# Maxout over expert-sorted rows: y tiles stored densely, gate and token number carried in the rows, output rows scattered

## Chip, cores and metric

The kernel runs on one core of one Trainium2 chip. The metric is device time in microseconds. Before the change the median of three runs is 1018.04 us (1016.11 to 1018.49); the profiled execution took 1017.2 us.

## The reference

Three stages in a row, all in float32. N = 3072 tokens (4 sequences of 768), width 512.

```python
# 1: attention, 8 heads of 64: window of 128 keys and 4 sink keys
a = softmax(where(keep, q @ k.T / 8, -1e9));  x = a @ v      # -> (3072, 512)
# 2: mixture of 8 experts, each token goes to one
logits = x @ w_gate + modality_bias[modality_id];  e = argmax(logits)
gate = softmax(logits)[e]
x = gate * (maximum(x @ w1[e], 0) @ w2[e])                   # 512 -> 1024 -> 512
# 3: Maxout layer
h = maximum(maximum(x @ w1, x @ w2), x @ w3)                 # 512 -> 768
out = h @ w_out                                              # 768 -> 512
```

In these inputs three experts get tokens; sorted by expert they fill 26 tiles of 128 rows, the last of each expert partly.

## The kernel before

All products of the last two stages are made of three float32r matmuls: each operand is split in a high part (ScalarE, a copy with rounding) and a low part (VectorE, original minus high), and `product` sums hi*hi, hi*lo and lo*hi.

**Attention** (up to 235 us) goes over 96 units of one head pair and 128 queries. GpSimd's part is `spread_sinks` and, for each finished sequence, `scatter`: six indirect DMAs that write 128 rows of `x_rows` each to `x_sorted`, at the position `pos` of the token among its expert's rows. `choose_gate` leaves the token's gate in a tile `gate` that stays to the end. Between the loads of q, k and v the SP queue also loads the first expert's weights, the Maxout weights, and zeroes the part of `y_sorted` behind row 3072.

**Tables** (240 to 262 us). From the counts VectorE works out which expert is where: `tab_i` row 0 says from which row of `x_sorted` tile j is read, row 1 whether it needs new weights. SP writes 128 zero rows behind each expert's last row. Between and after these steps VectorE makes `w1_lo`, the first `xT_lo`, and `pos_out`, the row of each token in `y_sorted`, where tile j lies at row 128 j. GpSimd waits for `pos_out_ready` before its loop.

**Expert stage** (257 to 593 us) runs over pairs of tiles, 24.5 us a pair, in one loop with 16 iterations, of which 13 do work. TensorE: `up` (hidden layer of a tile), `turn_h` (transposes), `turn_x` (transposes of the next x tile), `down`. ScalarE: `keep_xT`, `split_w1`, `split_w2`, `keep_h`, `keep_hT`, then `store_y` for both tiles, which issues the store of 128 rows on ScalarE's own queue. VectorE: the same tiles' low parts, and `keep_y`, which copies the result from PSUM to `y`. GpSimd loads the next x tiles (`load_x`). SP loads the second and third expert's weights when the first ones are split.

**Hand-over.** VectorE counts `experts_done` up after the loop; GpSimd waits for all stores (`stored`), and then gathers group 0 and 1 with eight indirect DMAs, one for each 128 tokens, through `pos_out`. A group is four tiles of 128 tokens. Meanwhile VectorE and ScalarE split Maxout weights (`split_m`, six slices of 128 columns; the first two were begun on ScalarE in the attention stage).

**Maxout stage** (611 us to the end), six groups of 67 us each. VectorE multiplies the gathered rows by the gate (`scale_y`); TensorE transposes them into PSUM (`turn_y`, banks `Y_BANK`); ScalarE and VectorE make `yT_hi` and `yT_lo` (`keep_yT`). `maxout(g)` makes 36 matmuls for each of six slices f, three results of 128 columns by 512 tokens, in two sets of banks; ScalarE and VectorE take the maximum, and a set is free for slice f + 2 when `g_kept` says so. `project(g)` makes four output tiles; ScalarE copies each to `o_sb`, and SP stores it to its place in `out`. The next group's tiles are transposed between `maxout` and `project`. A gather of group g + 2 starts when the tiles of group g are transposed.

The hand-over as GpSimd and TensorE see it:

```python
            pool.wait_ge(y_stored, stored)
            ...
            gather(0, 0)
            gather(1, 1)
```

Of the kernel before, what the change touches and what calls it, by code (L numbers as in the profile page):

```python
# [18 lines left out]
def build_program(nc, q_t, k_t, v_p, v_s, dims, n_sink, window, modality_id, w_gate, modality_bias, w1, w2,  # L19
# [25 lines left out]
    Y_BANK = (2, 3, 4, 1)  # L45

    x_sorted = nc.dram_tensor("x_sorted", (E * CAP, DM), F32, kind="Internal").ap()
    y_sorted = nc.dram_tensor("y_sorted", (TMAX * P, DM), F32, kind="Internal").ap()

    ctx = ExitStack()  # L50
    with ctx:
# [11 lines left out]
        pos_out = sb(ctx, "pos_out", [P, NT], I32)  # L63
        gate = sb(ctx, "gate", [P, NT])
        tab_i = sb(ctx, "tab_i", [P, 2, TW], I32)
# [7 lines left out]
        shift = sb(ctx, "shift", [P, E])  # L73
        moved = sb(ctx, "moved", [P, NT, E])
        pos_y = sb(ctx, "pos_y", [P, NT])
        onehots = sb(ctx, "onehots", [P, B, QT, E])
        zeros = sb(ctx, "zeros", [P, DM])
# [39 lines left out]
        x_rows = sb(one, "x_rows", [P, 2, QT, DM])  # L117
# [21 lines left out]
        near_i = sb(one, "near_i", [P, 1], I32)  # L139
        all_keys = sb(one, "all_keys", [P, S])  # L140
# [12 lines left out]

        cnt = sb(one, "cnt", [P, E])
# [16 lines left out]
        tab_f = sb(one, "tab_f", [P, 2, TW])  # L171
# [15 lines left out]
        y = [sb(two, f"y{i}", [P, DM]) for i in range(2)]  # L187
# [7 lines left out]
        yr = [sb(three, f"yr{i}", [P, GT, DM]) for i in range(2)]  # L195
# [43 lines left out]
        pos_out_ready, y_zeroed = sem("pos_out_ready"), sem("y_zeroed")  # L239
# [12 lines left out]
        results_there, o_free = sem("results_there"), sem("o_free")  # L252

        gathered = [sem(f"gathered{i}") for i in range(2)]
        m_hi_made, m_lo_made = sem("m_hi_made"), sem("m_lo_made")
        gated, y_turned, yT_hi_made, yT_lo_made = sem("gated"), sem("y_turned"), sem("yT_hi_made"), sem("yT_lo_made")
# [28 lines left out]
        def _(sp):  # L285
# [26 lines left out]
            assert len(between) == PAIRS - 2  # L312

            for g in range(2, PAIRS):
                sp.wait_ge(qk_free, g - 1)
                load_qk(g)
                sp.wait_ge(values_done, QT * (g - 1))
                load_v(g)
                dst, src, loaded = between[g - 2]
                sp.dma_start(dst, src).then_inc(loaded, 16)  # L320

            sp.wait_ge(counts_ready, 1)
            for e in range(E):
# [1152 lines left out]
```

## Time and profile before

| | before |
|---|---|
| median of three runs | 1018.04 us |
| profiled execution, its own time | 1017.2 us |
| its span, first to last instruction | 1015.6 us |
| TensorE busy | 945.2 us, 93% of the span |
| VectorE, ScalarE, GpSimd busy | 408.6, 310.2, 95.3 us |
| mean granted TensorE clock | 0.975 of full |
| one Maxout group, from one group's transposes to the next | 67.06 us |
| pitch of the matmuls of 512 columns there | 0.227 us |
| TensorE starts up(0,1), the second tile's first product | 265.60 us |
| y_sorted, one store, issue to landing | 2.0 us |

Times inside the profile count from the start of the span. An engine's name with a q behind it (ACTq, POOLq) is its sequencer, and the DMAs that it issues. The chain is the chain of work that ended last, followed back from the last instruction. The clock column tells the share of TensorE's full clock that was granted in a stretch.

### The profile page before, as it was taken

The numbers are of one execution on the slowest core, as the hardware profiler recorded it, in microseconds if no ns is written. First come the engines' busy times: TensorE is split into PE (matmuls) and PEld (weight loads), VectorE is DVE, ScalarE is ACT, GpSimd is POOL, SyncE is SP. The second block draws the span as 40 slices with busy tenths as digits, with TensorE's granted clock in tenths as the row PEclk, the third lists the DMA queues.
The fourth block names the chain that finished last, engine by engine and source line by source line (L and its number), as shares of the span: only waits on it lengthen the run. The fifth ranks groups of instructions, "written<-read, shape, count | busy, mean of one in ns | idle before, by whom it ended". The sixth has DMA issues, their size and how long they took to land.

```text
span 1015.6 us, 15686 instructions
## 1 busy us (share of the span) xinstructions
PE 945.2 (93%) x5166; PEld 757.7 (75%) x5166; DVE 408.6 (40%) x1308; ACT 310.2 (31%) x755; POOL 95.3 (9%) x175
## 2 busy tenths in 40 slices
PE   3999999991899999899999939999999999999998
PEld 2777776771788888678888737888888888888887
DVE  4778786866622222442222465312313223123120
ACT  2677676763311111321111333121211211112111
POOL 2111313132000000000000031010100100000000
PEclk9999999995899999999999979999999999999999
DMA  4455646534511111331111031020110200100001
GB/s 102 141 180 171 215 163 225 173 123 157 207 42 45 48 41 41 114 116 49 41 41 41 31 94 51 1 84 1 38 45 0 72 10 0 41 1 11 32 1 42
DMA packets 35987, 76.99 MB, mean 76 GB/s; under 512 B 7520, under 2 KB 9568, under 8 KB 35936
## 3 DMA queue, kind: packets, MB, share of 16 engines
q1 hardware_dynamic: 22048, 49.55, 14.3%
q0 software_dynamic: 6080, 19.93, 6.4%
q10 hardware_dynamic: 7808, 6.87, 2.1%
q8 instruction: 27, 0.44, 0.2%
q14 instruction: 24, 0.20, 0.1%
HBM read 52.74 MB, written 23.59 MB: 75 GB/s over the span
## 4 chain that ended last, share of the span: by engine, by line
PE 92%; DVE 4%; DMA 1%; issue 1%; ACT 1%; POOL 0%; DVEq 0%; ACTq 0%; POOLq 0%
PE bank L627 23%; PE bank L629 22%; PE bank L628 22%; PE bank L482 5%; PE bank L524 5%; PE bank L494 5%; PE bank L501 2%; PE bank L654 2%; PE bank L513 2%; PE bank L698 1%; PE bank L622 1%; DMA limits_i<-in_window 1%; DVE w_lo L1265 0%; DVE masked L991 0%; DVE w_lo L1311 0%
## 5 line engine op out<-in xcount | busy, mean ns | idle before, releaser
L629 PE MATMUL bank<-yT_hi,m_lo 128*128 128x512 f32 x432 | 168.3, 390 | 0.0
L756 ACT ACTIVATE probs<-masked,row_min 128x264 f32<-128x264 f32 (+1 forms) x192 | 93.4, 487 | 77.6 <-DVE row_min L991 77.6
L627 PE MATMUL bank<-yT_hi,m_hi_b 128*128 128x512 f32 x288 | 112.2, 390 | 0.0
L628 PE MATMUL bank<-yT_lo,m_hi_b 128*128 128x512 f32 x288 | 112.2, 390 | 0.0
L1397 DVE TENSOR_TENSOR b_sb<-bank,a_sb 128x512 f32<-128x512 f32 x36 | 24.9, 691 | 187.7 <-PE bank L629 187.7
L629 PEld LDWEIGHTS bank<-yT_hi,m_lo 128*128 128x128 f32 x432 | 81.1, 188 | 16.8
L627 PE MATMUL bank<-w_hi,xT_hi 128*128 128x512 f32 x208 | 84.7, 407 | 9.3 <-DVE w_lo L1265 5.0
L627 PE MATMUL bank<-w_hi,hT_hi 128*128 128x512 f32 x208 | 83.3, 400 | 5.1 <-DVE w_lo L1265 5.1
L915 ACT ACTIVATE gT_hi<-g_sb 128x512 fp32r<-128x512 f32 x36 | 22.8, 632 | 200.1 <-DVE g_sb L1400 200.1
L629 PE MATMUL bank<-w_hi,xT_lo 128*128 128x512 f32 x208 | 83.0, 399 | 0.0
L628 PE MATMUL bank<-w_lo,xT_hi 128*128 128x512 f32 x208 | 82.7, 398 | 0.0
L991 DVE CUSTOM_DVE_ANT_0 masked<-bank,masks 128x264 f32<-128x264 f32 (+1 forms) x192 | 70.5, 405 | 28.1 <-PE bank L482 27.1
L629 PE MATMUL bank<-w_hi,hT_lo 128*128 128x512 f32 x208 | 81.6, 393 | 0.0
L628 PE MATMUL bank<-w_lo,hT_hi 128*128 128x512 f32 x208 | 81.6, 392 | 0.0
L482 PE MATMUL bank<-kT,qT 64*128 64x264 f32 (+2 forms) x384 | 67.0, 428 | 12.0 <-issue 11.6
L869 ACT ACTIVATE xT_hi<-bank 128x512 fp32r<-128x512 f32 x27 | 16.6, 614 | 185.8 <-PE bank L622 185.8
L494 PE MATMUL bank<-ident,probs 128*128 128x128 f32 x352 | 61.1, 294 | 4.2 <-ACT probs L756 4.2
L628 PEld LDWEIGHTS bank<-yT_lo,m_hi_b 128*128 128x128 f32 x288 | 54.1, 188 | 11.2
L627 PEld LDWEIGHTS bank<-yT_hi,m_hi_b 128*128 128x128 f32 x288 | 54.1, 188 | 11.1
L524 PE MATMUL bank<-pT,v_in 128*64 128x128 f32 x704 | 60.4, 289 | 0.0
L524 PEld LDWEIGHTS bank<-pT,v_in 128*64 128x64 f32 x704 | 36.9, 137 | 29.5 <-issue 21.7
L627 PE MATMUL bank<-yT_hi,m_hi_a 128*128 128x512 f32 x144 | 56.2, 390 | 1.4 <-DVE yT_lo L1376 1.4
(189 smaller groups left out, 1562.5 us busy)
## 6 DMA issues: line engine op xcount, KB each, us to landing
w_sb<-in_moe_w SPq DMA_DIRECT2D x4, 2048.0 KB, 9.2
xr<-x_sorted POOLq DMA_DIRECT2D x28, 256.0 KB, 3.0
y_sorted<-y ACTq DMA_DIRECT2D x26, 256.0 KB, 2.0
kT<-in_k_t SPq DMA_DIRECT2D x16, 400.0 KB, 4.1
qT<-in_q_t SPq DMA_DIRECT2D x16, 384.0 KB, 3.4
v_in<-in_v_p SPq DMA_DIRECT2D x16, 384.0 KB, 2.9
out<-o_sb SPq DMA_DIRECT2D x24, 256.0 KB, 2.0
m_sb<-in_moe_w SPq DMA_DIRECT2D x6, 768.0 KB, 6.3
```

The costliest lines, as they stand in the source:

```text
L482: pe.matmul(bank[2 * (n % 2) + hd][:, 0:win_of(t)], qT[g % 2][rows, t * P:(t + 1) * P], kT[g % 2][rows, win_at(t):win_at(t) + win_of(t)], ...
L494: mm = pe.transpose(bank[(4, 7)[n % 2]][:, col:col + P], probs[n % 2][:, hd, at:at + P], ident[:, :])
L501: pe.matmul(bank[5][:, 0:PW], oT[n % 2][:, :], to_rows[:, n // QT % PPB, :], start=True, stop=True).then_inc(rows_ready, 1)
L513: pe.matmul(bank[6][:, 0:P], v_sink[g % 2][:, :], sink_cols[n % 2][:, :, :].rearrange("p a c -> p (a c)"), start=True, stop=False, skip_gr ...
L524: mm = pe.matmul(bank[6][D * hd:D * hd + D, 0:P], v_in[g % 2][:, tile, D * hd:D * hd + D], pT[n % 2][:, col:col + P], start=t < 2 and w == ...
L627: pe.matmul(psum, a_hi, b_hi, start=first, stop=False)
L628: pe.matmul(psum, a_hi, b_lo, start=False, stop=False)
L629: return pe.matmul(psum, a_lo, b_hi, start=False, stop=last)
L756: last = act.activation(probs[n % 2][:, hd, 0:win_of(t)], masked[n % 2][:, hd, 0:win_of(t)], ACT.Exp, bias=row_min[:, n % 2, hd:hd + 1], s ...
L915: act.activation(gT_hi[:, f, :], g_sb[:, f % 2, :], ACT.Copy).then_inc(gT_hi_made, 1)
L991: dve.tensor_tensor_reduce(out=masked[n % 2][:, hd, 0:win_of(t)], in0=bank[2 * (n % 2) + hd][:, 0:win_of(t)], in1=masks[:, min(t, 2), 0:wi ...
L1397: dve.tensor_tensor(b_sb[:, f % 2, :], bank[b0 + 1][:, :], a_sb[:, f % 2, :], ALU.max).then_inc(b_kept, 1)
```

## The change

- `keep_y` multiplies by the gate as it takes the result out of PSUM, so `scale_y` goes.
- Every row of `x_sorted` and `y_sorted` grows from 512 to 514 numbers; the last two are the gate and the token number. They are put into `x_rows` by `choose_gate` and by an iota of GpSimd, travel with the row, and come into `y` by a small load of its own, `load_meta`.
- `store_y` writes tile j at the row where the expert's rows really begin, so that experts follow each other without gaps; the zero rows at an expert's end are overwritten by the next expert's first tile, and therefore a store waits for the one before it. `tab_i` gets a third row with these starts, ready with `y_rows_ready`, for which ScalarE and GpSimd wait before their loops. `pos_out` and the zeroing of `y_sorted` go.
- The Maxout stage takes the rows in sorted order, 512 to a group, by plain loads on SP (`load_y`). Group 0 is loaded as soon as 12 tiles are stored, into `yr_first`, which no longer shares memory with expert tiles, and transposed into banks 4, 5, 6, 1.
- Output tiles are written by 24 indirect DMAs on GpSimd, to the rows that the token numbers name.
- At the hand-over `keep_yT(0)` comes first on ScalarE and behind one slice of `split_m` on VectorE; before, two and four slices came first.

```diff
-            for c in range(2):
-                at = slice((NT + c * (TMAX - NT) // 2) * P, (NT + (c + 1) * (TMAX - NT) // 2) * P)
-                between.append((y_sorted[at, :].rearrange("(t p) d -> p t d", p=P),
-                                zeros[:, None, :].broadcast_to([P, (TMAX - NT) // 2, DM]), y_zeroed))
...
-            def store(g):
-                for t in range(GT):
-                    sp.wait_ge(o_kept, GT * g + t + 2)
-                    sp.dma_start(out[bass.ds((GT * g + t) * P, P), :], o_sb[:, t, :]).then_inc(out_stored, 16)
...
+            def load_y(g):
+                sp.dma_start(yr[g % 2][:, :, :], y_sorted[g * GN:(g + 1) * GN, 0:DM].rearrange("(t p) d -> p t d", p=P)
+                             ).then_inc(y_loaded[g % 2], 16)
+
+            sp.wait_ge(y_stored, 16 * FIRST_TILES + 1)
+            load_y(0)
+            sp.wait_ge(results_there, 1)
+            sp.wait_ge(experts_done, 1)
+            load_y(1)
+            sp.dma_start(token[:, :, :], y_sorted[0:N, DM:XW].bitcast(I32).rearrange("(t p) o -> p t o", p=P)
+                         ).then_inc(token_loaded, 16)
+            for g in range(2, G):
+
+                sp.wait_ge(y_turned, GT * (g - 1))
+                load_y(g)
...
+            def name_tokens(b):
+
+                if b >= 2:
+                    pool.wait_ge(x_scattered, 16 * QT * (b - 1))
+                step(pool.iota(x_rows[:, b % 2, :, TOKEN].bitcast(I32), pattern=[[P, QT]], base=b * S, channel_multiplier=1))
...
+            def load_meta(j, par):
+                row = pool.value_load(tab_i[0:1, 0, bass.ds(j, 1)], min_val=0, max_val=E * CAP - P)
+                pool.dma_start(y[par][:, DM:XW],
+                               x_sorted[bass.ds(row, P), DM:XW]).then_inc(meta_loaded[par], 16)
...
+                    pool.wait_ge(y_stored, 32 * i + 1)
+                    for par in range(2):
+                        load_meta(2 * i + par, par)
...
-            gather(0, 0)
-            gather(1, 1)
...
+            pool.wait_ge(token_loaded, 16)
+            for g in range(G):
                 for t in range(GT):
+                    j = GT * g + t
+                    pool.wait_ge(o_kept, j + 2)
                     pool.indirect_dma_start(
+                        out=out[:, :], out_offset=bass.IndirectOffsetOnAxis(ap=token[:, j, TOKEN - DM:TOKEN - DM + 1], axis=0),
+                        in_=o_sb[:, t, :], in_offset=None).then_inc(out_stored, 16)
+                if g < G - 1:
+                    pool.wait_ge(out_stored, 16 * GT * (g + 1))
+                    pool.sem_inc(o_free, 1)
...
+            def turn_y(g, par, uses, last_g):
+                pe.wait_ge(y_loaded[par], 16 * uses)
+                banks = Y_BANK if last_g is not None else FIRST_BANK
                 for t in range(GT):
-                    pe.wait_ge(gated, GT * g + t + 1)
...
             def store_y(j, par):
+                row = act.value_load(tab_i[0:1, 2, bass.ds(j, 1)], min_val=0, max_val=N)
                 act.wait_ge(y_kept, j + 2)
-                act.dma_start(y_sorted[bass.ds(j * P, P), :], y[par][:, :]).then_inc(y_stored, 16)
+
+                act.wait_ge(y_stored, 16 * j + 1)
+                act.dma_start(y_sorted[bass.ds(row, P), :], y[par][:, :]).then_inc(y_stored, 16)
...
-            act.wait_ge(y_zeroed, 32)
             keep_xT(0, 0)
+            act.wait_ge(y_rows_ready, 1)
             with act.Fori(0, TMAX // 2) as i:
...
             act.wait_ge(experts_done, 1)
-            for f in range(2, 4):
-                split_m(f)
-            keep_yT(0)
-            for f in range(4, F3C):
+            keep_yT(0, FIRST_BANK)
+            for f in range(2, F3C):
                 split_m(f)
...
-                dve.wait_ge(y_stored, 32 * i + 1)
-                dve.tensor_copy(y[par][:, :], bank[out_bank][:, :]).then_inc(y_kept, 1)
+                dve.wait_ge(meta_loaded[par], 16 * i + 16)
+                dve.tensor_scalar(y[par][:, 0:DM], bank[out_bank][:, :], y[par][:, GATE:GATE + 1], None, ALU.mult
+                                  ).then_inc(y_kept, 1)
...
-            step(dve.tensor_scalar(shift[:, :], base[:, :], -1.0, None, ALU.mult))
-            step(dve.tensor_tensor(moved[:, :, :], onehots[:, :, :, :].rearrange("p b t e -> p (b t) e"),
-                                   shift[:, None, :].broadcast_to([P, NT, E]), ALU.mult))
-            step(dve.tensor_reduce(pos_y[:, :], moved[:, :, :], AX.X, ALU.add))
-            dve.tensor_tensor(pos_out[:, :], pos_y[:, :], pos[:, :], ALU.add).then_inc(pos_out_ready, 1)
+            step(dve.tensor_tensor(less_t[:, :, :], less[:, :, :], cnt[:, None, :].broadcast_to([P, E, E]), ALU.mult))
+            step(dve.tensor_reduce(first_y[:, :], less_t[:, :, :], AX.X, ALU.add))
+            step(dve.tensor_scalar(base[:, :], t_start[:, :], float(-P), None, ALU.mult))
+            step(dve.tensor_tensor(base[:, :], base[:, :], first_y[:, :], ALU.add))
+            step(dve.tensor_scalar(tm_b[:, :, :], cl, float(P), None, ALU.mult))
+            step(dve.tensor_tensor(tm_b[:, :, :], tm_b[:, :, :], by_expert(base), ALU.add))
+            step(dve.tensor_tensor(tm_b[:, :, :], tm_b[:, :, :], tm_a[:, :, :], ALU.mult))
+            step(dve.tensor_reduce(tab_f[:, 2, :], tm_b[:, :, :], AX.X, ALU.add))
+            dve.tensor_copy(tab_i[:, 2, :], tab_f[:, 2, :]).then_inc(y_rows_ready, 1)
...
-            for f in range(4):
-                split_m(f)
-            scale_y(0, 0, 0)
-            keep_yT(0)
-            for f in range(4, F3C):
+            split_m(0)
+            keep_yT(0, FIRST_BANK)
+            for f in range(1, F3C):
                 split_m(f)
```

## Rows read from the trace of the kernel before

**Rows 1.** Waits of TensorE from 240 us: line, releaser, total us, times, longest.
```profile
PE bank L698 <- DVE yr L1369: 13.3, 1, 13.3
...
PE bank L627 <- DVE w_lo L1265: 10.1, 4, 2.6
```

**Rows 2.** Chain that ended last, at the hand-over: start us, us, what.
```profile
592.98 0.70 DVE y L1305
...
593.86 2.03 DMA y_sorted<-y
...
596.76 1.51 POOL yr L460
...
602.13 3.53 DMA yr<-y_sorted,pos_out
...
611.32 0.50 PE bank L627
```

**Rows 3.** Timeline at the hand-over: start us, us, what [idle before it].
```profile
591.82 2.37 ACTq L883 DMA_DIRECT2D y_sorted<-y  x2
...
594.90 3.70 DVE L1362 TENSOR_TENSOR m_lo<-m_sb,m_hi_a 128x512 fp32r<-128x512 f32 x6 [1.23 <-issue]
596.20 3.23 ACT L833 ACTIVATE m_hi_b<-m_sb 128x512 fp32r<-128x512 f32 x6 [7.50 <-issue]
```

**Rows 4.** Timeline of ScalarE and VectorE at group 1's tiles.
```profile
661.87 2.04 ACT L909 ACTIVATE yT_hi<-bank 128x512 fp32r<-128x512 f32 x4
...
662.61 2.47 DVE L1376 TENSOR_TENSOR yT_lo<-bank,yT_hi 128x512 fp32r<-128x512 f32 x4
```

**Rows 5.** Windows: us, busy and count of PE, PEld, DVE, ACT, POOL; clock, DMA.
```profile
592.97:596.79 3.82, 0.00 (x0) 0.00 (x0) 2.58 (x5) 0.59 (x2) 0.03 (x1) 1.00 0.30 110
...
606.23:610.40 4.17, 3.67 (x16) 3.27 (x16) 3.20 (x6) 2.25 (x4) 2.02 (x3) 0.50 0.70 199
610.50:611.30 0.80, 0.00 (x0) 0.00 (x0) 0.69 (x1) 0.80 (x3) 0.62 (x1) 1.00 0.02 5
```

**Rows 6.** Windows in the expert loop, around TensorE's wait for w2_lo.
```profile
586.00:588.00 2.00, 0.75 (x3) 0.68 (x4) 2.00 (x2) 2.00 (x3) 0.00 (x0) 1.00 0.00 0
```

**Rows 7.** The last output tile (timeline), and the tile out.
```profile
1012.20 0.60 ACT L930 ACTIVATE o_sb<-bank 128x512 f32<-128x512 f32 x1 [3.48 <-PE bank L629]
...
L342 SPq DMA_DIRECT2D out<-o_sb x24: 332/332/372, 667.3 to 1013.0; - x24
...
DMA to landing us min/median/max: 2.0/2.0/3.9
```

**Rows 8.** Indirect DMAs: yr (640 to 730), x_sorted, and GpSimd's timeline.
```profile
DMA to landing us min/median/max: 3.3/3.5/4.4
...
L418 POOL DMA_INDIRECT x_sorted<-x_rows,pos x6: 960/961/1007, 237.4 to 243.8; - x6
...
248.00 0.59 POOL L434 DMA_DIRECT2D xr<-x_sorted  x1 [3.22 <-DMA x_sorted<-x_rows,pos]
```

**Rows 9.** Timeline, last table steps and start of the expert stage.
```profile
246.63 0.44 DVE L1239 TENSOR_REDUCE tab_f<-tm_b 128x34 f32<-128x272 f32 x1
...
260.05 0.18 DVE L1337 TENSOR_TENSOR pos_out<-pos_y,pos 128x24 int32<-128x24 f32 x1
...
263.05 0.60 ACT L869 ACTIVATE xT_hi<-bank 128x512 fp32r<-128x512 f32 x1 [9.40 <-PE bank L622]
...
264.30 0.54 POOL L441 DMA_DIRECT2D xr<-x_sorted  x1 [1.37 <-issue]
```

**Rows 10.** DMA issues: KB, us to landing; ScalarE's timeline over a pair's end.
```profile
y_sorted<-y ACTq DMA_DIRECT2D x26, 256.0 KB, 2.0
...
mod_i<-in_moe_modality_id ACTq DMA_DIRECT2D x1, 24.0 KB, 7.9
...
279.88 5.70 ACTq L883 DMA_DIRECT2D y_sorted<-y  x2
288.42 0.60 ACT L869 ACTIVATE xT_hi<-bank 128x512 fp32r<-128x512 f32 x1 [14.19 <-PE bank L622]
```

More of the change, by code:

```diff
@@ L62, in build_program @@
         pos = sb(ctx, "pos", [P, NT], I32)
-        pos_out = sb(ctx, "pos_out", [P, NT], I32)
-        gate = sb(ctx, "gate", [P, NT])
-        tab_i = sb(ctx, "tab_i", [P, 2, TW], I32)
+        token = sb(ctx, "token", [P, NT, XW - DM], I32)
+        tab_i = sb(ctx, "tab_i", [P, 3, TW], I32)
         rank_i = sb(ctx, "rank_i", [P, E], I32)
@@ L139, in build_program @@
         near_i = sb(one, "near_i", [P, 1], I32)
+        spare = sb(one, "spare", [P, 1792])
+        zeros = sb(one, "zeros", [P, XW])
         all_keys = sb(one, "all_keys", [P, S])
@@ L152, in build_program @@
         wide.close()
+        first_y = sb(one, "first_y", [P, E])
         cnt = sb(one, "cnt", [P, E])
@@ L186, in build_program @@
         hT_lo = [sb(two, f"hT_lo{i}", [P, F], F32R) for i in range(2)]
-        y = [sb(two, f"y{i}", [P, DM]) for i in range(2)]
+        y = [sb(two, f"y{i}", [P, XW]) for i in range(2)]
+        yr_first = sb(two, "yr_first", [P, GT, DM])
         two.close()
@@ L194, in build_program @@
         mo_hi = sb(three, "mo_hi", [P, F3C, DM], F32R)
-        yr = [sb(three, f"yr{i}", [P, GT, DM]) for i in range(2)]
+        yr = [yr_first, sb(three, "yr_second", [P, GT, DM])]
         yT_hi = sb(three, "yT_hi", [P, KC, GN], F32R)
@@ L697, in turn_y @@
                     for c in range(KC):
-                        mm = pe.transpose(bank[Y_BANK[t]][:, c * P:(c + 1) * P], yr[par][:, t, c * P:(c + 1) * P], ident[:, :])
+                        mm = pe.transpose(bank[banks[t]][:, c * P:(c + 1) * P], yr[par][:, t, c * P:(c + 1) * P], ident[:, :])
                     mm.then_inc(y_turned, 1)
@@ L903, in _, with keep_yT @@
                         store_y(2 * i + par, par)
-            def keep_yT(g):
+            def keep_yT(g, banks):
                 for t in range(GT):
@@ L1363, in split_m, with keep_yT @@
                 last.then_inc(m_lo_made, 1)
-            def scale_y(g, par, i):
-                for t in range(GT):
-                    if t == 0:
-                        dve.wait_ge(gathered[par], 16 * GT * (i + 1))
-                    dve.tensor_scalar(yr[par][:, t, :], yr[par][:, t, :], gate[:, bass.ds(GT * g + t, 1)], None,
-                                      ALU.mult).then_inc(gated, 1)
-            def keep_yT(g):
+            def keep_yT(g, banks):
                 for t in range(GT):
@@ L1387, in _, with group @@
             dve.tensor_tensor(mo_lo[:, :, :], mo_sb[:, :, :], mo_hi[:, :, :].bitcast(F32), ALU.subtract).then_inc(m_lo_made, 1)
-            def group(g, par, i, last=False):
+            def group(g, last=False):
                 for f in range(F3C):
@@ L1403, in group @@
                                       ).then_inc(gT_lo_made, 1)
-                    if f == F3C - 3 and not last:
-                        scale_y(g + 1, 1 - par, i + par)
                 if not last:
-                    keep_yT(g + 1)
-            with dve.Fori(0, G // 2 - 1) as i:
-                group(2 * i, 0, i)
-                group(2 * i + 1, 1, i)
-            group(G - 2, 0, G // 2 - 1)
-            group(G - 1, 1, G // 2 - 1, last=True)
+                    keep_yT(g + 1, Y_BANK)
+            with dve.Fori(0, G - 1) as g:
+                group(g)
+            group(G - 1, last=True)
 _INS = ["n_sink", "window", "moe_modality_id", "moe_w_gate", "moe_modality_bias", "moe_w1", "moe_w2",
```

76 lines of the change are left out of this document (33 added, 43 removed).

## The prediction

> **What bounds the kernel now.** I read the waits of TensorE from 240 us on first [rows 1]. The reader is to see how few they are. After the attention stage the matrix engine waits for results in only a handful of places, and the largest single one, 13.3 us before the transposes of line 698, is the hand-over from the expert stage to the Maxout stage. Everywhere else the time is set by the number of matmuls, which this change leaves alone. So the change can win about what that hand-over costs, and lose only where it makes a new wait.
>
> The chain that ended last, followed through the hand-over [rows 2], says what the 13.3 us are made of. The last expert matmul has ended when VectorE copies y at 592.98 (to 593.67), the last y tile is stored (landed at 595.89), GpSimd starts the first of four indirect gathers at 596.76, and the fourth, started at 602.13, lands at 605.66. Then come the scaling by the gate, the 16 transposes (from 606.23, 3.67 us [rows 5]), one ScalarE copy and the last VectorE subtraction; the first Maxout matmul starts at 611.32. From the end of the last expert matmul to it: 18.3 us.
>
> The timeline of the same stretch [rows 3] shows what the other engines would be ready for. VectorE has left the expert loop at 594.90, ScalarE at 596.20. Both then do splits that the transposed tiles don't depend on.
>
> **The change at the hand-over.** Group 0's four y tiles now come by a plain load issued on SP once 12 tiles are stored, out of the 26 of this run. It waits behind the expert weights in SP's queue, but those are all issued 150 us before the hand-over, so the data is there. TensorE's 16 transposes need nothing else (banks 4, 5, 6, 1 are already read) and follow the last expert matmul at about 593; at the full clock they take half of their 3.67 us, so they end near 595. That they come early is no gain in itself, since the copies set the end: ScalarE does its first yT_hi copy where it now does its first split, 596.20. VectorE does split_m(0), three subtractions at 3.70/6 = 0.62 us, from 594.90 to 596.75, and then the four yT_lo. In the steady state four such copies take ScalarE 2.04 us and four subtractions take VectorE 2.47 us [rows 4]. With the first yT_hi ready at about 596.8, VectorE ends at 596.85 + 2.47 = 599.3 and the first Maxout matmul starts at 599.35. That is 611.32 - 599.35 = 12.0 us earlier. The gathers, the scaling by the gate and the landing of the last store lie off the path.
>
> ScalarE's start could move. A store now waits for the store before it: the one issued at 591.82 lands 2.0 us later [rows 3, 10], that is at 593.85, where the second store was issued anyway. I charge 0.1 us, so 11.9. From below VectorE's own order holds: it can't finish before 594.90 + 1.85 + 2.47 = 599.2, a gain of 12.1. From above, ScalarE spends 2.0 us between its last store and its first split, all of it issue; twice that gives a gain of 9.9.
>
> Is something late next? After 599.3 VectorE owes five splits (5 x 1.85) and the split of mo (about six chunks of 0.62, 3.7), so it is free at 612.3, and g_sb of the first f is kept at about 613.7. TensorE wants it for the third f, 72 matmuls at the steady pitch of 0.227 us after 599.35, at 615.7. It fits, with 2 us to spare.
>
> **The clock.** TensorE now stops twice instead of once. In the trace its clock is at the full level (2.4 GHz) for the first 3.8 us of idleness and at half (1.2 GHz) when it restarts at 606.23, and is at the full level again from 610.5 [rows 5]; the price fell on transposes, inside the wait. In the expert loop a wait of 2.6 us left the level at 1.00 [rows 1, 6]. After the change the idle stretch behind the early transposes is about 594.8 to 599.35, 4.5 us, longer than the one that kept the level and about as long as the one that had lost it. If the level falls, the first Maxout matmuls run at half rate, at most for the 4.2 us of [rows 5], which costs half of that, 2.1 us, and nothing if it holds. I take 1.7, since part of the half-rate stretch can lie in the idle time.
>
> A rule bears on this. In rows 5 nothing but transposes ran between 606.23 and 609.9, and the level rose right after them: transposes count. The Trainium skill, TensorE: Matmul & The Clock Gate, Part 4 (PE-mode transpose), says the opposite, that a transpose doesn't count as busy in the same way. By that rule the early transposes would not shorten the pause, the fall would be certain, and the cost the full 2.1 us in place of 1.7; by this case's rows it is less. It is a rival below.
>
> **The end.** Output rows leave by an indirect DMA on GpSimd instead of a plain store on SP. The last o_sb is kept at 1012.80, SP issues at 1013.0 and the rows land 2.0 us later at 1015.0, 0.6 before the end of the span [rows 7]. Now GpSimd takes 0.3 us to start, as between its gathers, and an indirect DMA lands 3.5 us after its issue in the quiet Maxout stage (3.3 to 4.4); at the end of the attention stage GpSimd waited 3.22 us for a scatter of such rows beyond the 0.96 us of issuing it [rows 8]. So 1012.80 + 0.3 + 3.5 = 1016.6 in place of 1015.0: +1.6 us. Bounds: +0.3 if it lands as a plain store does, 2.0 us after its start (nothing makes it faster than that), and +2.7 with the 4.4. The skill's page DMA: Bandwidth & Descriptors, Anatomy of one DMA, fits 2.0 us plus bytes over 436e3 for a DMA from GpSimd, an estimate of 2.6 us for 256 KB, by which the tail would be +0.7. The other 20 scatters are hidden: an output tile comes every 4.1 us (18 matmuls), a scatter occupies GpSimd for 1.0 us, and o_sb is wanted again only a group (67 us) later.
>
> **The start of the expert stage.** Four VectorE steps (259.07 to 260.23) become nine: four on the tile table, of which three like the one of 0.44 us, two of 64 elements and three short ones, together about 2.9 us instead of 1.16. y_rows_ready thus comes at 261.98, and ScalarE now waits for it before its loop. Behind that wait stand three register loads and the copy of the second x tile, which ran at 263.05 [rows 9]. A register load and the issue around it took GpSimd 1.37 us [rows 9]. If ScalarE's three overlap, it is ready at 263.5; if they don't, at 262.0 + 4.1 = 266.1, which is 3 us late. TensorE wants that tile's xT_lo only when up(0,1) starts, at 265.60, and VectorE makes it in 0.7 us after ScalarE's copy, by 264.4 in the trace, so 1.2 us of delay is free. Cost: 0 to 1.9 us; I take 0.3, as ScalarE's loads are short where it leaves the loop (2.0 us for everything, rows 3). VectorE's own extra 1.75 us is covered by its wait for the same copy; GpSimd's next x load comes 1.75 us later, with 8 us to spare before the transposes that read it.
>
> **Edits at nothing.** The metadata loads (one per tile, 8 bytes a row) are queued on GpSimd behind the next x loads; they are issued some 5 us into a pair, and needed when down(i,0) ends, 15 us later. Value for price: the modality numbers, 24 KB in pieces of the same 8 bytes, landed in 7.9 us [rows 10], and that is also the size of the token load, which is wanted 45 us after it is issued. Without that cover either would cost up to 7.9 us once (the token load) or the part past 15 us in each of 13 pairs. Multiplying y by the gate on its way out of PSUM has the shape of a VectorE operation that takes 0.69 us with an immediate factor, the same as the copy it replaces. The iota in the attention stage (at most 0.2 us, four times) lies in GpSimd's waits of over 2 us a unit. Rows of 2,056 bytes instead of 2,048 add 0.4% to hidden transfers. The zeroing of y_sorted and the four scalings in every group go; both were hidden, so they give nothing.
>
> **Sum.** -11.9 (hand-over) + 1.7 (clock) + 1.6 (last scatter) + 0.3 (entry) = -8.3 us. Against the profiled execution's 1017.2 us that is 1008.9. It lies 0.8 below the median of the runs, 1018.04; I lay the difference on the middle of the two, 1017.6, and get 1009.3. A measurement of this kernel can't tell changes within about 0.3% (3 us) from none.
>
> **Rivals.**
> - The clock holds through the second pause. For it: a 2.6 us wait did no harm and the early transposes cut the pause. Against: 4.5 us is nearer to the pause that lost it. 1009.3 - 1.7 = 1007.6 us. Chance 0.25.
> - Transposes don't count (the skill's rule above): a fall for certain and its full price, 1009.7 us. Against it stands the rise at 610.5. Chance 0.06.
> - A new wait takes part of the place: ScalarE reaches the first yT_hi up to 2 us later than 596.2 because its longer loop code has to be left, or the entry to the expert loop costs its 1.9 us. Each gives 1010.5 to 1011.5, both together 1013.3. Chance 0.12.
> - The load of group 0 is not early after all (behind SP's queue), so that its landing takes the place of the gathers: issue at 595.9, four tiles in about 6 us, the transposes at 602 and the matmuls at 607, 4 us of gain against 1.6 of tail and no change to be measured, 1015.5. Against it: SP's queue is empty 150 us earlier. Chance 0.03.
> - Slower: the wait in store_y. ScalarE now stands still until the store before has landed. It issues a pair's first store at 279.88 and is next wanted at 288.42 [rows 10]. With a landing of 2.0 us nothing happens; if the rows of 2,056 bytes, not aligned in memory, took more than 8.5 us, each further us would be paid in all 13 pairs. From 9.4 us on the kernel is slower by over 0.3%; at 10 us it takes 1009 + 13 x 1.5 = 1029 us. Only the size of the landing decides, and the slowest y store or gather around here took 4.4 us. Chance 0.04.
>
> **How the numbers follow.** The forecast (gain, clock falls) has 0.50, its own range 1008 to 1010.5. Faster by over 0.3%, that is below 1014.6 to 1015: 0.50 + 0.25 + 0.06 + 0.12 = 0.93 less 0.01 for a bad sum of upper ends: 0.92. Within 0.3%: 0.03 and that 0.01, 0.04. Slower: 0.04. The range takes in the rival with the clock held and a short tail (1007.6 - 1.3, 1006.3) and most of the new waits, up to 1012.5.
>
> **What the profile will show.** Right: the wait of line 698's successor before group 0 gone; 16 transposes straight behind the last expert matmul; the first Maxout matmul 6.4 us after it, not 18.3; a granted clock of 0.50 for up to 4 us there; the last scatter landing about 3.8 us after the last o_sb; the pairs of the expert loop as long as before (24.5 us). Wrong: TensorE waiting for y_loaded; VectorE waiting for the metadata; an entry to the expert loop later than 265.5 at the second tile; stores that land after more than 8 us.

## The result, and the profile after

| | before | after |
|---|---|---|
| median | 1017.09 us (4 runs, 1016.11 to 1018.49) | 1024.48 us (4 runs, 1023.57 to 1026.02) |
| profiled execution, its own time | 1017.2 us | 1023.57 us |
| its span | 1015.6 us | 1021.7 us |

The ratio is 1.0069 (95% interval 1.0051 to 1.0087): slower, 15 us above the forecast. In the two spans the 6.1 us divide so (my sums, from the start of one row to the start of another; a pair is the time from one `turn_h` to the next but one, two tiles):

| stretch | before | after | difference | forecast |
|---|---|---|---|---|
| start to first `up` | 257.27 | 258.83 | +1.6 | 0 |
| first `up` to first `turn_h` | 13.77 | 14.40 | +0.6 | +0.3 |
| the two pairs around the first change of expert | 57.90 | 62.49 | +4.6 | 0 |
| ten other pairs | 247.94 | 249.04 | +1.1 | 0 |
| last pair, to the last copy of y | 16.10 | 17.60 | +1.5 | 0 |
| hand-over, to the first Maxout matmul | 18.34 | 6.57 | -11.8 | -11.9 |
| Maxout stage, to the last `o_sb` | 400.88 | 402.28 | +1.4 | +1.7 |
| last `o_sb` to the end of the span | 3.4 | 10.5 | +7.1 | +1.6 |

The waits of TensorE from 240 us (line, releaser, total us, times, longest) answer to [rows 1]:

```profile
PE bank L640 <- DMA xr<-x_sorted: 16.1, 1, 16.1
PE bank L645 <- DVE w_lo L1285: 10.1, 4, 2.6
PE bank L645 <- DVE xT_lo L1307: 6.9, 3, 4.7
PE bank L645 <- DVE yT_lo L1394: 4.9, 1, 4.9
```

The 13.3 us before line 698 are gone. In their place stand 4.9 us for the first `yT_lo`, as forecast (4.5), and, not forecast, one wait of 4.7 us for an `xT_lo`: a new stall inside the expert loop.

The chain at the hand-over (start us, us, what), against [rows 2]:

```profile
602.36 0.76 DVE y L1325
603.37 2.41 DMA y_sorted<-y
605.78 0.60 ACT yT_hi L931
606.40 2.49 DVE yT_lo L1394 x4
608.93 0.79 PE bank L645
```

Behind the last y copy stand 2.7 us until ScalarE starts its first copy, this copy, and four subtractions: no gather, no scaling, no transpose. The chain puts 2.4 of the 2.7 us down to the landing of the last y store. That is an inference which the code doesn't bear out: ScalarE waits for the store before the last one, and for the last one only GpSimd waits. From the start of the y copy to the start of that ScalarE copy are 3.4 us here and 3.3 in e4_no_wait below, where ScalarE waits for no store; the prediction had 3.2, for leaving the loop.

The windows (columns as in [rows 5]), over the second half of the expert stage's last weight change, the pause, and the first Maxout matmuls:

```profile
594.00:599.00 5.00, 3.87 (x11) 3.08 (x12) 4.55 (x5) 2.57 (x3) 0.00 (x0) 0.66 0.00 0
...
606.00:608.50 2.50, 0.00 (x0) 0.00 (x0) 2.28 (x5) 2.50 (x6) 0.00 (x0) 1.00 0.23 17
608.50:611.90 3.40, 2.97 (x7) 2.39 (x8) 3.40 (x7) 3.40 (x8) 0.00 (x0) 0.50 1.05 300
612.00:614.00 2.00, 2.00 (x10) 1.67 (x9) 2.00 (x4) 2.00 (x5) 0.00 (x0) 1.00 0.89 131
```

The clock fell to its lower level at the first Maxout matmul, for the 3.4 us of the window, as the likeliest case had it. It also fell in the last pair (0.66 on average over 594 to 599), where [rows 6] had shown it unmoved.

The end, in the timeline, against [rows 7]:

```profile
1011.21 0.60 ACT L952 ACTIVATE o_sb<-bank 128x512 f32<-128x512 f32 x1 [3.48 <-PE bank L647]
1012.08 0.97 POOL L484 DMA_INDIRECT out<-o_sb,token  x1 [3.11 <-ACT o_sb L952]
```

The scatter starts 0.27 us after the copy and lands 2.7 us after its start (the median of the 24), at 1014.8. But the span goes on to 1021.7. What runs in those 7 us shows in the instructions of the program's last line, which every engine executes (duration ns, min/median/max, then first and last start):

```profile
L55 POOLq DRAIN  x1: 9611/9611/9611, 1011.8 to 1011.8; - x1
L55 SPq COMPARE_BRANCH  x1: 38/38/38, 1014.8 to 1014.8; - x1
L55 SPq DRAIN  x1: 7/7/7, 1015.0 to 1015.0; - x1
L55 SPq EVENT_SEMAPHORE  x1: 17/17/17, 1021.6 to 1021.6; - x1
```

SyncE has seen the last scatter land at 1014.8 and would be through at 1015. GpSimd's closing drain, 9.6 us from 1011.8 on, is what the other engines meet at 1021.5. In the kernel before, the same instruction took longer and cost nothing, since GpSimd's work ended with the gathers, 219 us before the end:

```profile
L51 POOLq DRAIN  x1: 11484/11484/11484, 796.5 to 796.5; - x1
```

In the view of waits SyncE's last 6.7 us are put down to another engine, which had long been done: the releaser named there is an inference, and the long instruction beside it is the cause.

The stall in the expert loop, ScalarE's timeline around 440 us, after:

```profile
431.62 3.90 ACT L870 ACTIVATE w_hi<-w_sb 128x1024 fp32r<-128x1024 f32 x4 [4.72 <-PE bank L647]
438.78 8.33 ACTq L905 DMA_DIRECT2D y_sorted<-y  x2
450.41 0.60 ACT L888 ACTIVATE xT_hi<-bank 128x512 fp32r<-128x512 f32 x1 [14.90 <-DMA y_sorted<-y]
```

and before:

```profile
437.51 4.00 ACTq L883 DMA_DIRECT2D y_sorted<-y  x2
444.42 0.60 ACT L869 ACTIVATE xT_hi<-bank 128x512 fp32r<-128x512 f32 x1 [10.04 <-PE bank L622]
```

Before, the pair's two stores were issued within 4.0 us and ScalarE waited for TensorE. After, the second store's issue ends 8.3 us after the first began, and the next `xT_hi` comes 11.6 us after the first store in place of 6.9. The first store is in flight while the next expert's weights arrive (two DMAs of 2 MB, on SP's queue from 421.66 on; the second is issued at 437.4 and lands at 447.8). It is the slowest y store of this trace, and it isn't slower than it was; the landings of all y stores, after and then before:

```profile
DMA to landing us min/median/max: 2.4/2.8/7.8
```

```profile
DMA to landing us min/median/max: 2.0/2.0/7.9
```

So the new wait makes the stall, and no new slowness of the store.

The table's 4.6 us for these two pairs are the net of two things. The pair with the stall takes 35.27 us, 6.2 more than before: 4.7 of waiting, and a fall of the clock behind it, at 451. The pair ahead of it takes 27.21 us, 1.6 less than before, since a fall of the clock that the trace of before has at 416 is missing here. Where the same stall meets a trace with that fall, in e1_sp_out below, the two pairs take 63.8 us, 5.9 more than before.

### The profile page after: what moved, and what is told of

The parts are those of the page before. It is cut to its first block, busy times and chain, and to the rows that moved or that the text cites. A ratio compares the mean times of both kernels' runs of the same rounds, so it can differ in the third digit from the quotient of the medians.

```text
span 1021.7 us, 15881 instructions
## 1 busy us (share of the span) xinstructions
PE 948.0 (93%) x5166; PEld 757.9 (74%) x5166; DVE 401.5 (39%) x1289; ACT 309.6 (30%) x755; POOL 108.5 (11%) x205
## 4 chain that ended last, share of the span: by engine, by line
PE 89%; DVE 4%; DMA 2%; issue 2%; ACT 1%; POOL 1%; ACTq 0%; POOLq 0%; DVEq 0%
PE bank L645 22%; PE bank L647 22%; PE bank L646 21%; PE bank L500 5%; PE bank L542 5%; PE bank L512 5%; PE bank L519 2%; PE bank L672 2%; PE bank L531 2%; DMA y_sorted<-y 1%; PE bank L640 1%; PE bank L717 1%; DMA limits_i<-in_window 1%; DVE w_lo L1285 1%; POOL x_sorted L430 1%
## 5 line engine op out<-in xcount | busy, mean ns | idle before, releaser
L645 PE MATMUL bank<-w_hi,xT_hi 128*128 128x512 f32 x208 | 85.1, 409 | 11.9 <-DVE xT_lo L1307 6.9
L500 PE MATMUL bank<-kT,qT 64*128 64x264 f32 (+2 forms) x384 | 67.3, 430 | 11.9 <-issue 11.6
L484 POOL DMA_INDIRECT out<-o_sb,token x24 | 23.3, 971 | 411.4 <-ACT o_sb L952 411.4
## 6 DMA issues: line engine op xcount, KB each, us to landing
xr<-x_sorted POOLq DMA_DIRECT2D x28, 256.0 KB, 3.0
```

Source lines behind the costliest of these rows:

```text
L484: pool.indirect_dma_start(out=out[:, :], out_offset=bass.IndirectOffsetOnAxis(ap=token[:, j, TOKEN - DM:TOKEN - DM + 1], axis=0), in_=o_sb ...
L500: pe.matmul(bank[2 * (n % 2) + hd][:, 0:win_of(t)], qT[g % 2][rows, t * P:(t + 1) * P], kT[g % 2][rows, win_at(t):win_at(t) + win_of(t)], ...
L645: pe.matmul(psum, a_hi, b_hi, start=first, stop=False)
```

## The experiments

Each is compared with the kernel before on the same chip. Two questions had the most at stake: what the last 7 us are, and what the expert loop lost.

**e1_sp_out: the output stores back on SP.**

```diff
+                for t in range(GT):
+                    sp.wait_ge(o_kept, GT * g + t + 2)
+                    sp.dma_start(out[(GT * g + t) * P:(GT * g + t + 1) * P, :], o_sb[:, t, :]).then_inc(out_stored, 16)
...
-                    pool.indirect_dma_start(
-                        out=out[:, :], out_offset=bass.IndirectOffsetOnAxis(ap=token[:, j, TOKEN - DM:TOKEN - DM + 1], axis=0),
-                        in_=o_sb[:, t, :], in_offset=None).then_inc(out_stored, 16)
```

> The changed kernel with its 24 output tiles stored by plain DMAs on SP, as before the change, in sorted order (so output rows stand in another order; all arithmetic is done). Theory A (GpSimd's closing DRAIN, which ran from 1011.85 to 1021.46 us in the changed kernel and from 796.5 to 808.0, hidden, in the kernel before, is exposed because GpSimd now issues the last DMA): the span ends about 2.8 us after the last o_sb instead of 9.9, 7 us less than the changed kernel, about 1017.4 us. Rival B (the scatters slow the Maxout stage, or land late): the drain stays as it is or the gain is spread over the six groups; B by landing alone would give back 14.8 - 15.0 = nothing, under 1 us.

Measured: 1017.58 us, ratio 1.0003 (0.9987 to 1.0019), against 1.0069 with the scatters. From the last `o_sb` (1010.61) to the end of the span (1013.5) are 2.9 us instead of 10.5. The drain is still there, just ahead of the Maxout stage and 400 us before the end:

```profile
L55 POOLq DRAIN  x1: 6441/6441/6441, 605.9 to 605.9; - x1
```

So the 7 us at the end belong to GpSimd being the last to work, and not to the landing of the rows.

**e2_late_plain: the kernel before, with one plain 256 KB store on GpSimd after the last output tile.**

```diff
+            pool.wait_ge(o_kept, NT + 1)
+            pool.dma_start(late_out[:, :], o_sb[:, GT - 1, :]).then_inc(late, 16)
```

> The kernel before the change, plus one plain 256 KB store that GpSimd issues after the last output tile is kept, into a scratch tensor. Theory A (any late DMA of GpSimd pulls the drain to the end): slower than the kernel before by about 6 to 7 us, 1023 to 1024 us, with a DRAIN of 8 to 10 us at the end of GpSimd's program. Rival B (it is peculiar to indirect DMAs): slower by 1 to 2 us only, for the landing of 3.0 in place of 2.0 us.

Measured: 1023.18 us, ratio 1.0072 (1.0055 to 1.0088). One plain store is enough to turn the kernel before into one as slow as the changed one. Its last `o_sb` is at 1012.74, and the last line's instructions are:

```profile
L53 POOLq DRAIN  x1: 6974/6974/6974, 1013.6 to 1013.6; - x1
L53 SPq DRAIN  x1: 7/7/7, 1016.6 to 1016.6; - x1
```

SyncE is done at 1016.6, the span ends at 1020.8. An indirect DMA is not needed for the price.

**e8_drain_early: the changed kernel with a drain of GpSimd before its last two scatters.**

```diff
+                    if j == NT - 2:
+                        pool.drain()
                     pool.wait_ge(o_kept, j + 2)
```

> The changed kernel with one explicit drain of GpSimd put before its last two scatters. In the first experiment the closing DRAIN took 6.4 us although GpSimd's last DMA lay some 20 us behind it. Theory A (a drain costs this fixed time whenever it is taken): the closing DRAIN still takes over 8 us and the time stays at 1024. Rival B (it clears up after all software DMAs since the last drain, and an early one leaves little): the closing DRAIN shrinks and the time falls by up to 5 us, to 1019.

Measured: 1023.07 us, ratio 1.0043 (1.0028 to 1.0058). The trace is of the fastest of the four runs, 1018.58 us (the others: 1023.00 to 1023.57), so only its rows at the end are used here, not its time. The closing drain shrank to 3.9 us, and ends with the landing of the last scatter. But the inserted one took its place:

```profile
L484 POOLq DRAIN  x1: 9447/9447/9447, 1002.1 to 1002.1; - x1
...
L55 POOLq DRAIN  x1: 3856/3856/3856, 1012.6 to 1012.6; - x1
```

The last two scatters, due at 1006.5 and 1010.5 by the pitch of 4.08 us, started at 1012.32 and 1013.60. So the long drain was paid once here, by whichever drain came first, and it should be free where GpSimd is idle for 9 us; e9_drain_group tests that.

**e4_no_wait: tiles of y at row 128 j, no wait for the store before.**

```diff
-                act.wait_ge(y_stored, 16 * j + 1)
...
-            step(dve.tensor_reduce(tab_f[:, 2, :], tm_b[:, :, :], AX.X, ALU.add))
+            step(dve.tensor_scalar(tab_f[:, 2, :], tile_no[:, :], float(P), None, ALU.mult))
```

> The changed kernel with each y tile stored at row 128 j, so that stores don't overlap and ScalarE doesn't wait for the store before; the register load of the row is kept. The Maxout stage then works on the first 24 stored tiles, padding included, and output tiles are scattered to consecutive rows, so the output is another one; the amount of work is the same. Theory A (the wait for the landing costs 4.7 us once): 4 to 5 us less than the changed kernel, about 1019.5. Rival B (it is the register load or ScalarE's longer loop): less than 1 us less.

Measured: 1015.67 us, ratio 0.9992 (0.9979 to 1.0006). The twelve intervals sum to 305.91 us, against 311.53 after and 305.84 before: the two pairs at the change of expert take 28.85 and 28.90 (27.21 and 35.28 after), the others, but for the last with its change of expert, 24.51 to 24.60 (24.63 to 24.69). A landing is as long as it was (2.4/2.7/7.8 us min/median/max), but nobody waits for it:

```profile
438.08 3.98 ACTq L904 DMA_DIRECT2D y_sorted<-y  x2
444.63 0.60 ACT L889 ACTIVATE xT_hi<-bank 128x512 fp32r<-128x512 f32 x1 [9.73 <-PE bank L641]
```

**e3_pool_store: the ordered stores on GpSimd, each landing waited for.**

```diff
+            def store_y(j, par):
+                row = pool.value_load(tab_i[0:1, 2, bass.ds(j, 1)], min_val=0, max_val=N)
+                pool.wait_ge(y_kept, j + 2)
+                pool.dma_start(y_sorted[bass.ds(row, P), :], y[par][:, :]).then_inc(y_stored, 16)
+                pool.wait_ge(y_stored, 16 * j + 16)
```

> The changed kernel with the ordered y stores issued, and waited for, by GpSimd instead of ScalarE, so that ScalarE never stands still for a landing and needs no row register. Theory A (the 9.4 us lost in the expert stage are 4.7 from the one store that met the second expert's weight load while ScalarE stood still, some 1 us from 0.1 a pair, 2.2 at the entry, 1.5 from a clock fall): 5 to 6 us less than the changed kernel, about 1018.5 us, and no wait of TensorE for xT_lo at the change of expert. Rival B (the wider rows or the metadata loads make the stage longer, whoever issues): the same time as the changed kernel, 1024.

Measured: 1018.59 us, ratio 1.0021 (1.0008 to 1.0034). The ordinary pairs fell to 24.47 us and the pairs of the change to 28.83 and 28.88, but the pair after the change took 26.6, because the wait for the landing now held GpSimd's next x load:

```profile
PE bank L646 <- DMA xr<-x_sorted: 16.8, 2, 14.9
```

Two waits, the first of 14.9 us at the entry, the other of 1.9. The stall had moved, and was smaller.

**e7_pool_store2: as e3_pool_store, with the second store's landing waited for only after the next x loads.**

```diff
+                if par:
+                    pool.wait_ge(y_stored, 16 * j)
+                pool.dma_start(y_sorted[bass.ds(row, P), :], y[par][:, :]).then_inc(y_stored, 16)
...
+                    with pool.If(i > 0):
+                        pool.wait_ge(y_stored, 32 * i)
```

> The full computation. GpSimd issues the y stores, as in the third experiment, but waits for a pair's last landing only behind the next x loads, so that the load of the x tile after a change of expert isn't late (it cost 1.9 us there). Theory A: the stage takes as long as before the change, 2 us less than the third experiment, about 1016.5 us, level with the kernel before. Rival B (GpSimd's program is too full, its loads are late anyway): 1018.5 again.

Measured: 1014.98 us, ratio 0.9957 (0.9942 to 0.9971); the whole computation, and faster than before. The same slow landing is there, in GpSimd's timeline, and delays nothing:

```profile
438.32 0.55 POOL L466 DMA_DIRECT2D y_sorted<-y  x1 [23.27 <-DVE y L1324]
447.15 0.55 POOL L466 DMA_DIRECT2D y_sorted<-y  x1 [8.29 <-DMA y_sorted<-y]
448.89 0.54 POOL L453 DMA_DIRECT2D xr<-x_sorted  x1 [1.19 <-issue]
```

The twelve intervals sum to 305.22 us, 6.3 less than after. 26 loads of metadata and the multiplication by the gate are in these 24.46 us pairs, so they cost nothing.

**e6_row64: rows of 528 numbers, 2,112 bytes (33 x 64), the changed kernel otherwise.**

```diff
-    XW = DM + 2
+    XW = DM + 16
```

> The changed kernel with rows of 528 numbers (2112 bytes, a multiple of 64) in place of 514 (2056): 16 numbers of metadata instead of 2. Rival B (rows that begin off a multiple of 64 bytes land more slowly): a y store lands in 2.0 to 2.2 us again instead of 2.8, and GpSimd waits 3.2 us for the last scatter of the attention stage instead of 4.4 to 6.1; the time falls by 1 to 3 us against the changed kernel (1024.5). Theory A (the row width hardly matters, the order of the stores does): landings as in the changed kernel and the same time within 1.5 us.

Measured: 1023.95 us, ratio 1.0043 (1.0029 to 1.0057). The DMA issues (KB each, median us to landing), of the changed kernel and of this one:

```profile
y_sorted<-y ACTq DMA_DIRECT2D x26, 257.0 KB, 2.8
```

```profile
y_sorted<-y ACTq DMA_DIRECT2D x26, 264.0 KB, 2.1
```

More bytes, and 0.7 us less: the row length was behind the slower landing, and behind the longer wait for the last x scatter too (2.96 us here, 4.4 to 6.1 in the ten traces with rows of 2,056 bytes, 3.22 in [rows 8]). The slowest landing stayed (7.6 us), and with it the stall (36.15 us for that pair). So the alignment is real, and isn't what made the kernel slow.

**e5_both: the edits of e1_sp_out and e4_no_wait together.**

> The changed kernel with both edits of the first two experiments on it: plain output stores on SP in sorted order, and y tiles stored at row 128 j with no wait for the store before (so the output is another one; the work is the same). Theory A (the closing drain and the ordered store are all that the forecast missed): the forecast's own time, 1009.3 us, between 1007.5 and 1011; the two gains of 6.9 and 8.8 us add up only in part, since about 1.5 us of the second was a clock fall that some executions have and others don't. Rival B (the rest of the change costs something more that these two hid): above 1012.

Measured: 1007.66 us (6 runs, 1005.76 to 1011.65), ratio 0.9892 (0.9874 to 0.9911). With plain output stores the forecast's 1.6 us for the last scatter fall away too, so the forecast for this kernel is -8.3 - 1.6 = -9.9 us, a ratio of 0.9903: inside the interval. Without the two faults the change is worth what the forecast gave it.

**e9_drain_group and e11_after_drain_group: one drain ahead of the last group**, where GpSimd is idle for 52 us, in e7_pool_store2 and in the changed kernel.

```diff
+                    if j == NT - GT:
+                        pool.drain()
                     pool.wait_ge(o_kept, j + 2)
```

> The full computation, e7_pool_store2 with one drain of GpSimd ahead of the last group of Maxout, where e7's GpSimd stood idle for tens of us. Theory (the closing drain costs what GpSimd's transfers since its last drain have left to clear away): the closing drain falls from 9.8 us to about 4, as in e8_drain_early, and since this drain stands in idle time it holds no scatter: the tail after the last o_sb falls from about 10.5 to 5 us, and the time is 4 to 6 us below e7's ratio of 0.9957, so about 0.990 to 0.992 of before. Rival (a drain costs its full length wherever the last transfer is near): closing drain still near 9 us, time as e7, ratio 0.996. A third: the early drain reaches into the last group and holds its first scatters, which shows as later rows of o_sb in the last group and a ratio near 1.

> The full computation, the changed kernel with one drain of GpSimd ahead of the last group of Maxout and nothing else. Theory: the tail falls from 9.7 to about 5 us and nothing else moves, so some 4.5 us below the changed kernel's 1024.5: about 1020, ratio near 1.002 to 1.003. Rival (the closing drain costs its full length again): 1024, ratio 1.007.

Measured: e9_drain_group 1008.54 us, ratio 0.9893 (0.9876 to 0.9909); e11_after_drain_group 1016.19 us, ratio 0.9971 (0.9958 to 0.9985). Both gained more than expected. Of e9_drain_group the two drains, and the last scatters in GpSimd's timeline:

```profile
L495 POOLq DRAIN  x1: 8237/8237/8237, 941.9 to 941.9; - x1
...
L55 POOLq DRAIN  x1: 3153/3153/3153, 1004.1 to 1004.1; - x1
```

```profile
992.10 0.97 POOL L497 DMA_INDIRECT out<-o_sb,token  x1 [52.07 <-ACT o_sb L953]
996.18 0.97 POOL L497 DMA_INDIRECT out<-o_sb,token  x1 [3.11 <-ACT o_sb L953]
1000.26 0.97 POOL L497 DMA_INDIRECT out<-o_sb,token  x1 [3.11 <-ACT o_sb L953]
1004.34 0.97 POOL L497 DMA_INDIRECT out<-o_sb,token  x1 [3.11 <-ACT o_sb L953]
```

The closing drain now ends at 1007.3, within 0.3 us of the landing of the last scatter (1004.34 + 2.7); no scatter is late. From the last `o_sb` to the end are 4.0 us in both kernels. That is 6.5 us less than after, and it is the price of the undrained end. Between the spans of the changed kernel and e11_after_drain_group (1021.7 and 1013.3) lie 8.4 us: these 6.5, and 2.1 by which the first `up` happened to start earlier (256.77 against 258.83), less 0.2 of small things. By the two ratios the gain is 10 us, but the kernel before took 1019.48 us in this round and 1017.09 in the first one, so ratios of the two rounds don't compare to better than some 2 us. What the traces show of the drain is the 6.5.

**e10_split_early: e9_drain_group, with VectorE's first `split_m` ahead of the expert loop.**

```diff
+            split_m(0)
 
             with dve.Fori(0, TMAX // 2) as i:
...
-            split_m(0)
             keep_yT(0, FIRST_BANK)
```

> The full computation, e9_drain_group with the three subtractions of the first Maxout matrix (m_lo of f = 0) moved from after the expert loop on VectorE to before it. Theory: the hand-over from the last y copy to the first turn_y loses about 1.9 us (three subtractions of about 0.64 us), and the clock either falls as before or not: ratio 0.2 to 0.4 per cent below e9's. Rival (PE waits there for the rows of y_sorted, loaded back, and not for m_lo): hand-over unchanged, time as e9's. A third: the early subtractions wait for the Maxout weights and delay the first xT split, which shows as a later first up.

Measured: 1007.54 us, ratio 0.9881 (0.9865 to 0.9898); against e9_drain_group the intervals overlap, but the trace shows the gain. The hand-over falls from 6.27 to 5.03 us, 1.2 and not 1.9, since another thing is late next, ScalarE's first copy:

```profile
597.21 2.07 ACT L932 ACTIVATE yT_hi<-bank 128x512 fp32r<-128x512 f32 x4 [7.76 <-DVEq L1390]
597.84 2.48 DVE L1397 TENSOR_TENSOR yT_lo<-bank,yT_hi 128x512 fp32r<-128x512 f32 x4 [1.74 <-ACT yT_hi L932]
```

ScalarE waits for VectorE to have left its loop (`experts_done`), 1.9 us after the start of the last y copy. The Maxout stage takes 402.53 us, no less than with the longer pause: the clock still falls.

## Why the prediction was wrong

**The hand-over: right, size and reason.** -11.8 us, forecast -11.9. The first Maxout matmul starts 6.6 us after the last y copy, and it waits for the four `yT_lo`, in the order that was worked out.

**The clock at the first Maxout matmul: right.** +1.4 us, forecast +1.7; in the eleven traces of the changed kernel and its variants the Maxout stage takes 402.3 to 402.8 us, against 400.88. The rival in which the clock holds is refuted, and in e10_split_early a fall came behind a pause of 3.3 us too. The rival in which transposes don't count has the fall as well; its full price of 2.1 us was not reached in any of the eleven, but whether transposes count could not be told from these runs.

**The end: this step failed.** The prediction put it as "1012.80 + 0.3 + 3.5 = 1016.6 in place of 1015.0: +1.6 us". The landing was in fact shorter, 2.7 us. By the Trainium skill, DMA: Bandwidth & Descriptors, Anatomy of one DMA, the estimate was 2.6 us, and the trace agrees. (The two bounds are 0.2 too high by their own terms: 1012.80 + 0.3 + 2.0 and + 4.4 give +0.1 and +2.5.) What failed is the silent step behind it, that the span ends when the last rows have landed. It was so only as long as GpSimd's drain was over before. Moving the last DMA to GpSimd put its closing drain at the end of the path, 5.5 us more than was charged. The row was in the trace of before, 11.5 us long at 796.5, and wasn't priced because nothing waited for it. e1_sp_out, e2_late_plain and e11_after_drain_group each show it alone: without it, with it in the other kernel, and paid early.

**The wait in `store_y`: this step failed.** The prediction charged it 0.1 us at the hand-over, and made it a rival only if the landing took more than 8.5 us in all 13 pairs. No y store took that long. The slowest landed in 7.8 us, and the wait cost 4.7 us there, with a fall of the clock behind it 6.2. Two things were wrong. The 8.5 us were read from one ordinary pair, as the time from the first store to the next `xT_hi`; at the change of expert this time is 6.9 us before. And the landing isn't all that must fit into it: the second store is issued only behind it, and from there to `xT_hi` pass 3.8 us. 7.8 + 3.8 - 6.9 = 4.7 us, which is the wait that TensorE shows. In the other ten pairs the wait cost 0.11 us each, 1.1 us together, where the prediction had said that nothing happens. [rows 10] gave the median landing, 2.0 us, and the text took 4.4 us for the slowest around; that same trace has a y store of 7.9 us, at 437.51, and a wait meets the slowest. e4_no_wait takes both costs away by itself (305.91 us), and e7_pool_store2 does it with the wait kept, on an engine with time to spare.

**The entry: right.** From the first `up` to the first `turn_h` the six traces in which ScalarE doesn't wait for `y_rows_ready` (before, and the kernels whose stores are on GpSimd among them) take 13.73 to 14.27 us, 13.95 on average, the seven in which it does 14.14 to 14.42, 14.36 on average: 0.4 us, forecast 0.3. The pair of traces in the table above gives 0.6, and chance is in it.

**Edits at nothing: right.** The metadata and token loads, the multiplication by the gate (0.75 us where the copy took 0.70) and the zero rows stood beside pairs of 24.46 us in e7_pool_store2, no longer than before (24.49 to 24.60). Rows of 2,056 bytes were not only 0.4% longer: they land 0.7 us later. It is hidden.

**The profiled execution of before was a lucky one in the last pair.** It shows 16.10 us from the last `turn_h` to the last y copy; each of the other twelve traces, e2_late_plain among them, whose expert stage is that of before, shows 17.4 to 17.8. [rows 6] was read as "a wait of 2.6 us left the level at 1.00". In the other traces that same wait was followed by a fall, worth 1.5 us. The reading was partial besides: the 10.1 us of [rows 1] are four such waits, and behind two of them the clock of that same trace did fall, at 416 and 433. The window around the second, before:

```profile
430.00:436.00 6.00, 3.44 (x9) 2.48 (x8) 4.43 (x4) 3.90 (x4) 0.00 (x0) 0.74 0.00 0
```

Over all 13 traces 38 of the 52 waits of 2.5 to 2.6 us have such a fall, by their place in the program 10, 13, 3 and 12 of 13. So of the +6.1 us in the spans the 1.5 us in the last pair are no effect of the change, and no error of the forecast; the 1.6 us by which the pair ahead of the stall is shorter aren't either, and the two cancel.

**What is left.** The forecast was 14.4 us below the span of after (1015.6 - 8.3 = 1007.3 against 1021.7): 5.5 the end, 4.6 the two pairs at the change of expert (6.2 the stall, less the 1.6 just named), 1.1 the other pairs, 1.5 the clock in the last pair, 0.3 the entry, -0.2 the hand-over and the clock together, and 1.6 in the first `up` starting later. The last one stays open: in the traces with the changed tables that start lies anywhere between 256.0 and 258.8 us. Of the 1.6 us 1.2 lie in the attention stage: the last x scatter starts at 245.01 us after and at 243.79 before, and in the thirteen traces anywhere from 243.3 to 245.0. From there on the chain of the trace after runs through the 6.1 us of waiting for that scatter, whose slower landing (e6_row64) may have made the rest; that wasn't separated.

## What to carry to other kernels

Before the last DMA of a kernel is moved to another engine, look at what that engine's closing instructions cost in the trace of before, hidden or not; a drain of GpSimd in an idle stretch ahead of the last transfers takes most of that price away. A wait for a landing, put on an engine that feeds the critical path, is to be priced by the slowest landing of that transfer, not by its median, and against the time that is free at that very place, less what the engine still has to do behind the landing. One profiled execution is one draw: a short fall of the clock behind a wait may be in it or not.

## What the runs showed of the hardware

- A closing drain of GpSimd took 6.4 to 11.5 us wherever it came first after GpSimd's DMAs. With another drain 62 us ahead and four scatters between, it took 3.2 us and ended with the last landing. What sets the 6.4, 7.0, 9.6 or 11.5 us of the first one wasn't separated.
- A store of 128 rows of 2,056 bytes landed in 2.8 us (median), of 2,112 bytes in 2.1, of 2,048 bytes in 2.0.
- The y store of 256 KB that is in flight together with a 2 MB load of weights took 7.6 to 8.1 us to land in all thirteen traces, 7.9 in the kernel before; the median of the y stores is 2.0 to 3.0.
- TensorE's clock fell to its lower level (1.2 GHz) also after a pause of 3.3 us, in e10_split_early not at the restart but 1.4 us behind it, and in or right behind 38 of 52 waits of 2.5 to 2.6 us. Where traces with and without such a fall can be compared, it cost 1.5 to 1.6 us.
